# Expert routing in a fused attention, dense layer and mixture-of-experts kernel: choice, ranks and slot lists built in groups of four token tiles

## What is computed

```python
# 1. attention, 4 batches x 8 heads, 576 x 64, half the heads with a local mask, half with a strided one
attn = softmax(mask(q @ k.T / 8)) @ v
# 2. a dense layer, 512 -> 1024 -> 512
h = x @ w_in
solu = h * softmax(h)
x2 = (layer_norm(solu) * g_ln) @ w_out
# 3. top-1 mixture of 8 experts, 512 -> 1024 -> 512
logits = x2 @ w_gate + modality_bias[modality_id]
e_idx = argmax(logits, axis=1)                 # one expert per token
gate_w = softmax(logits)[arange(N), e_idx]
for e in range(8):
    mask = e_idx == e
    out[mask] = gate_w[mask, None] * (relu(x2[mask] @ w1[e]) @ w2[e])
```

## Time and profile before

| | us |
|---|---|
| median of 3 executions | 636.38 |
| lowest, highest | 634.66, 639.98 |
| the profiled execution, its own time | 635.12 |
| its span, first to last instruction | 633.4 |
| granted TensorE clock, mean | 0.995 |

### The profile page before, as it was taken

The page is one execution under the profiler, slowest core; times in us unless marked ns, Lnnn a source line. Parts: engine busy times, 40 slices in busy tenths (PEclk is TensorE's granted clock), DMA queues, the critical chain, the costliest instruction groups (busy, mean ns, idle before and its releaser), DMA issues.

```text
span 633.4 us, 12550 instructions
## 1 busy us (share of the span) xinstructions
PE 607.4 (96%) x3794; PEld 505.3 (80%) x3795; DVE 359.4 (57%) x1032; ACT 242.1 (38%) x775; POOL 205.6 (32%) x242
## 2 busy tenths in 40 slices
PE   4999999989999999999999998999999998999995
PEld 3677776768888888888888897998998976788994
DVE  5899999766787888888888954231211200021210
ACT  3788888824233333334344322212222211112210
POOL 5555555530333433455554434110011011101001
PEclk9999999999999999999999999999999998999999
DMA  8877667100000070000000000010870035000000
GB/s 184 177 170 166 159 161 176 49 0 18 18 32 18 17 283 17 17 33 17 17 17 17 18 34 1 31 37 21 303 275 17 31 120 215 17 15 31 0 30 33
DMA packets 70861, 47.35 MB, mean 75 GB/s; under 512 B 56728, under 2 KB 58744, under 8 KB 70832
## 3 DMA queue, kind: packets, MB, share of 16 engines
q1 hardware_dynamic: 68832, 41.21, 22.9%
q0 software_dynamic: 2000, 5.77, 2.5%
HBM read 37.40 MB, written 10.22 MB: 75 GB/s over the span
## 4 chain that ended last, share of the span: by engine, by line
PE 77%; issue 8%; POOL 7%; DMA 2%; DVE 2%; SPq 2%; ACT 1%; POOLq 0%; DVEq 0%; ACTq 0%
PE bank L571 16%; PE bank L997 16%; PE pair L982 16%; PE pair L571 15%; POOL work L543 4%; PE pair L1521 3%; PE pair L1090 2%; POOL w_lo L550 2%; PE pair L1511 2%; PE pair L1117 2%; PE bank L1110 1%; DMA xT<-x_dram,g_idx 1%; SPq L415 1%; DMA arena<-in_k 1%; PE pair L692 1%
## 5 line engine op out<-in xcount | busy, mean ns | idle before, releaser
L982 PE MATMUL pair<-x_hi,lead_hi 128*128 128x256 f32 x288 | 82.2, 285 | 0.2 <-DVE lead_h L1042 0.2
L982 PE MATMUL pair<-x_lo,lead_hi 128*128 128x256 f32 x288 | 81.5, 283 | 0.0
L982 PE MATMUL pair<-x_hi,lead_lo 128*128 128x256 f32 x288 | 81.5, 283 | 0.0
L1053 POOL DMA_INDIRECT out<-work,lead_sidx x18 | 18.0, 998 | 165.4 <-ACT work L1037 159.4
L763 ACT ACTIVATE work<-pair,neg_max 96x128 f32<-96x128 f32 (+2 forms) x176 | 61.6, 368 | 18.7 <-PE bank L703 14.8
L543 POOL TENSOR_TENSOR work<-work,row_inv 96x512 f32<-96x512 f32 (+3 forms) x48 | 44.8, 933 | 54.4 <-DVE row_inv L850 54.4
L1042 DVE SCALAR_TENSOR_TENSOR lead_h<-pair,lead_h 128x512 fp32r<-128x512 f32 x18 | 12.4, 691 | 86.7 <-ACT lead_h L1030 86.5
L1432 POOL TENSOR_TENSOR rstd<-ln_small 128x1 f32 (+1 forms) x18 | 26.5, 1472 | 107.2 <-DVE ln_small L638 107.2
L571 PE MATMUL bank<-w_hi,lnT_hi 128*128 128x512 f32 x144 | 58.5, 406 | 1.1 <-DVE lnT_lo L1269 1.1
L571 PE MATMUL pair<-w_hi,x_hi 128*128 128x512 f32 x144 | 58.3, 405 | 0.2 <-ACT arena L752 0.2
L571 PE MATMUL bank<-w_hi,lnT_lo 128*128 128x512 f32 x144 | 56.7, 393 | 0.0
(11 more groups left out here) (209 smaller groups left out, 1393.2 us busy)
## 6 DMA issues: line engine op xcount, KB each, us to landing
entry<-in_moe_w SPq DMA_DIRECT2D x12, 1024.0 KB, 9.3
arena<-in_q SPq DMA_DIRECT2D x32, 144.0 KB, 2.9
arena<-in_k SPq DMA_DIRECT2D x32, 144.0 KB, 3.4
x_dram<-work SPq DMA_DIRECT2D x18, 256.0 KB, 2.0
arena<-in_moe_w SPq DMA_DIRECT2D x8, 512.0 KB, 7.1
arena<-in_v SPq DMA_DIRECT2D x16, 144.0 KB, 2.6
work<-in_v SPq DMA_DIRECT2D x16, 135.0 KB
arena<-in_moe_w_in SPq DMA_DIRECT2D x8, 256.0 KB, 3.2
```

What stands on the lines that cost most here:

```text
L982: ins = pe.matmul(lead_h_ps[n % 2][:, jj * BLK:(jj + 1) * BLK], a[:, w], b[:, x], start=(passes == 1), stop=(passes == 3 * KC))
L1053: pool.indirect_dma_start(out=out, out_offset=bass.IndirectOffsetOnAxis(ap=lead_sidx[:, tt:tt + 1], axis=0), in_=lead_y[tt], in_offset=Non ...
```

## The change

The routing no longer runs tile by tile. The gate weights become the stationary operand: each of the four 128-row chunks of `w_gate` is padded with zeros to 32 columns and writes its partial logits to its own 32 rows of one PSUM bank, with up to 512 tokens (four tiles, `GROUPED`) moving. ScalarE copies the bank, TensorE transposes it back tile by tile, and one VectorE reduction adds the four partial sums. Group 0 (tiles 0 to 3) is done in slot 6, for the choice of the leader; groups 1 to 4 are all done in slots NT and NT+1. Choice, exponentials and gates are done for all tiles of a phase at once, and the ranks with two matmuls and a scan. The inverse is no longer a matmul: the rank gives a row of a table in DRAM, POOL writes (token, gate) pairs there with 18 indirect DMAs of 8 bytes per token, and SP's seven copies read from the table. The second copy of the transposed x2 (`x2_T`), `spread`, `invert_slots`, `add_slots` and the count matmul are gone. The slots end at NT+1.

```diff
-        wg = sb("wg", KC * E)
+        wg = sb("wg", KC * STRIDE)
...
+        slot_tab = nc.dram_tensor("slot_tab", [E * T, 2], F32)
...
@@ attention_sp, behind the four constant loads
+            sp.wait_ge(consts, 3)
+            sp.dma_start(slot_tab.rearrange("(p n) w -> p (n w)", p=P), zeros).then_inc(tab_zeroed, 16)
...
@@ attention_dve
+            dve.memset(wg[:, :], 0.0)
...
-        LAST = NT + 3
+        LAST = NT + 2
...
+        GROUPED = [range(g, min(g + SNAP, NT)) for g in range(0, NT, SNAP)]
...
@@ solu_pe
+            def gate_logits(g):
+                first, n = group_cols(g)
+                pe.wait_ge(x2T_kept, GROUPED[g][-1] + 1)
+                wait(pe, lgT_out, g)
+                if g == 1:
+                    pe.wait_ge(lead_chosen, 1)
                 for c in range(KC):
+                    rows = slice(c * STRIDE, (c + 1) * STRIDE)
+                    ins = pe.matmul(lgT_ps[rows, 0:n], wg[:, rows], xT[:, c * T + first:c * T + first + n],
+                                    start=True, stop=True, skip_group_check=True)
+                ins.then_inc(lgT_ready, 1)
+
+            def turn_logits(g):
+                pe.wait_ge(lgT_out, g + 1)
+                wait(pe, lg_taken, g)
+                for k in range(len(GROUPED[g])):
+                    ins = pe.transpose(lg_ps[:, k * P:(k + 1) * P], lgT[:, k * P:(k + 1) * P], ident[:, :])
+                ins.then_inc(lg_turned, 1)
...
+            def ranks():
+                pe.wait_ge(hot_ready, 2)
+                pe.matmul(lgT_ps[:, 0:NE], before[:, :], hot[:, :], start=True, stop=True)
+                pe.matmul(lgT_ps[:, NE:2 * NE], ones_bf[:, :], hot[:, :], start=True, stop=True,
+                          skip_group_check=True).then_inc(rank_ready, 1)
 
             def slot(t):
                 if at(t, NT):
                     lead_up(pe, 0, 0)
-                    ranks(t - 3)
+                    gate_logits(1)
                     turn_x2(t - 2)
                     turn_ln(t - 1)
                     lead_up(pe, 0, 1)
-                    logits(t - 2)
+                    turn_logits(1)
+                    gate_logits(2)
                     down(t - 1, 0)
-                    invert_slots(t - 3)
+                    turn_logits(2)
+                    gate_logits(3)
                     down(t - 1, 1)
                     return
                 if at(t, NT + 1):
                     lead_up(pe, 0, 2)
-                    ranks(t - 3)
+                    turn_logits(3)
                     turn_x2(t - 2)
                     lead_up(pe, 0, 3)
-                    logits(t - 2)
-                    return
-                if at(t, NT + 2):
-                    ranks(t - 3)
+                    gate_logits(4)
                     lead_down(pe, 0, 0)
-                    invert_slots(t - 4)
+                    turn_logits(4)
                     lead_down(pe, 0, 1)
-                    invert_slots(t - 3)
+                    ranks()
                     return
...
@@ solu_act
             def take_x2T(t):
                 act.wait_ge(x2_turned, t + 1)
-                wait(act, lg_ready, t)
-                act.copy(x2_T, x2T_ps[:, :]).then_inc(x2T_out, 1)
                 act.copy(xT[:, :]...
...
@@ solu_dve, behind the slots; place() is twelve small operations on 128x18 to 128x144 elements
             lead_rest_x(dve, 1, 1)
-            add_slots(NT - 2)
-            add_slots(NT - 1)
-            lead_block_dve(dve, 1)
+            gates(2, SNAP, NT)
+            for n in range(4):
+                lead_rest_h(dve, 1, n)
+            lead_stage_scatter(dve, 1)
+            place()
+            lead_rest_x(dve, 2, 0)
+            lead_rest_x(dve, 2, 1)
...
@@ solu_pool
             def slot(t):
-                if inside(t, 3):
-                    spread(pool, t - 3)
...
             lead_block_pool(pool, 0)
             lead_block_pool(pool, 1)
+
+            pool.wait_ge(tab_zeroed, 16)
+            pool.wait_ge(tab_idx_ready, 1)
+            for t in range(NT):
+                pause(pool)
+                pool.indirect_dma_start(out=slot_tab, out_offset=bass.IndirectOffsetOnAxis(ap=tab_idx[:, t:t + 1], axis=0),
+                                        in_=tok_pair[:, 2 * t:2 * t + 2], in_offset=None).then_inc(tab_written, 16)
...
@@ experts_sp
             sp.wait_ge(meta_ready, 1)
+            sp.wait_ge(tab_written, 16 * NT)
             with sp.Fori(0, E - 1) as k:
...
-                sp.dma_start(slots[:, :].rearrange("p (i n) -> p i n", i=2)[:, :, bass.ds(first, NT)],
-                             inv[:, 0:2 * E * NT].rearrange("p (i n) -> p i n", i=2)[:, :, bass.ds(e * NT, NT)]
-                             ).then_inc(slots_ready, 16)
+                sp.dma_start(slots[:, bass.ds(2 * first, 2 * NT)],
+                             slot_tab.rearrange("(e p n) w -> e p (n w)", e=E, p=P)[bass.ds(e, 1)]
+                             .rearrange("o p m -> (o p) m")).then_inc(slots_ready, 16)
```

More of the change, by code:

```diff
@@ L162, in fused_kernel @@
         first_w = sb("first_w", E)
[L163 to L177, removed]
+        iota_e = sb("iota_e", E)
+        NE = E * NT
+        rt = sb("rt", 5 * NE)
+        lgs, lg_exp, eq_w, run_n, rank_of = (rt[:, i * NE:(i + 1) * NE] for i in range(5))
+        by_te = lambda x: x.rearrange("p (t e) -> p t e", e=E)
+        by_et = lambda x: x.rearrange("p (e t) -> p e t", e=E)
+        hot = sb("hot", NE, BF16)
+        not_first = sb("not_first", NE)
+        tok_f = sb("tok_f", 5 * NT)
+        l_max, sum8, rank_f, row_base, rank_hi = (tok_f[:, i * NT:(i + 1) * NT] for i in range(5))
+        rank_i = sb("rank_i", 2 * NT, I32)
+        tab_idx = sb("tab_idx", NT, I32)
+        zeros = rt[:, 0:2 * E * T // P]
         n_f = sb("n_f", 2 * E)
@@ L895, in slots_of @@
                 body(t)
-            with eng.Fori(3, SNAP + 3) as t:
+            with eng.Fori(3, SNAP + 2) as t:
                 body(t)
-            for t in range(SNAP + 3, FIRST_PIECE):
+            for t in range(SNAP + 2, FIRST_PIECE):
                 body(t)
@@ new lines, in turn_logits, with count_snap @@
+            def turn_logits(g):
[4 more added lines that the diff above has]
+                ins.then_inc(lg_turned, 1)
+            def count_snap():
+                pe.wait_ge(hot_ready, 1)
+                pe.matmul(lgT_ps[:, 0:E * SNAP], ones_bf[:, :], by_et(hot[:, :])[:, :, 0:SNAP],
+                          start=True, stop=True).then_inc(snap_ready, 1)
@@ L1165, in slot @@
                     up_tile(pe, t, 0)
-                if inside(t, 3):
-                    ranks(t - 3)
+                if at(t, SNAP + 2):
+                    gate_logits(0)
+                if at(t, SNAP + 3):
+                    count_snap()
                 if inside(t, 2):
@@ L1171, in slot @@
                     turn_ln(t - 1)
+                if at(t, SNAP + 2):
+                    turn_logits(0)
                 if not (static(t) and t < 2):
                     up_tile(pe, t, 1)
-                if inside(t, 2):
-                    logits(t - 2)
                 if inside(t, 1):
                     down(t - 1, 0)
-                if inside(t, 3):
-                    invert_slots(t - 3)
-                if inside(t, 1):
                     down(t - 1, 1)
@@ L1330, in slot @@
                     lead_rest_h(dve, 0, 1)
+                    take_logits(1)
+                    take_logits(2)
                 if at(t, NT + 1):
+                    take_logits(3)
                     lead_rest_h(dve, 0, 3)
+                    take_logits(4)
+                    choose(2, SNAP, NT)
                 if inside(t, 0):
```

242 lines of the change are left out of this document (116 added, 126 removed).

## The result

The changed kernel takes 640.44 us (median of 20, 637.22 to 641.92) where the kernel before takes 636.75 (median of 20, 634.66 to 640.33). The ratio is 1.0048, with a 95% interval from 1.0031 to 1.0066: slower by half a per cent. The forecast was 620.0 with a range to 627.5, so it was wrong by 20 us and on the wrong side. The profiled execution has a span of 637.5 us, against 633.4.

What follows compares the result with a forecast made beforehand. TensorE, busy 96% of the span, was taken as the bound. From 635.12 us, 23.2 of removed work went and 7.6 of added came, making 619.5; half of 1.26 on top gave 620.0, range 615.0 to 627.5.

Steps and rivals of the forecast that it cites:

- The slot lists: POOL and SP queues: 18 indirect writes at 1.29 us each and seven copies, all hidden with 1.4 us slack.
- the sum: Whole kernel: 635.12 - 23.2 + 7.6 = 619.5 us, plus half of 1.26 gives 620.0.
- Rival 4: `turn(0)`, block 5: slot table too late; chance 0.08 still faster, 0.04 slower than before; 643.8 at 2.7 us each.
- Column groups: `gate_logits` on TensorE: four matmuls work at the same time, 1.06 us a full group, 0.63 the last, 4.9 together.
- Rivals 1 and 2: `gate_logits`: overlap only in part, 2.15 us a group, 625.8, chance 0.20; no overlap, 3.44, 631.6, chance 0.08.
- rival 1: `gate_logits`: records start in program order, so only neighbours overlap; 2.15 us a group, 625.8 in all; chance 0.20.
- turn_logits: Added on TensorE: 18 transposes back, at 0.49 us for four, 2.2 us together.
- ranks and counts: Added on TensorE: `ranks` and `count_snap` once, three small bf16 matmuls, 0.2 us.
- waits: TensorE's new waits for ScalarE's bank copies and VectorE's operations, mostly covered by other work: 0.3 us.
- At the start: Ahead of attention's loop: a small VectorE memset and one more DMA, taken as 0, upper bound 3.9 us.
- Is TensorE still last?: Solu slots: each shrinks by 1.18 to 12.37 us; low part of x keeps a slack of 0.45, so TensorE stays last.
- Rival 3: Solu slots: VectorE's chain sets the slot, each gives back some 0.2 us, 2.8 together, 622.8; chance 0.12.

Runs made afterwards that it cites:

- group 3: Changed kernel untouched, 622.74 us, and with three edits that do nearly nothing, 624.58, 622.69 and 622.63; the kernel before beside them, 635.34.
- the five groups: The sets in which all follow-up kernels ran, each on one chip at one time with its own runs of the kernel before; 622.63 to 656.28 us.
- both groups: Changed kernel without its 18 indirect writes, in two sets of runs: 623.03 us (ratio 0.9755) and 623.02 us (ratio 0.9782).
- the dummies of group 1: Kernel before plus 18 indirect DMAs behind block 1's scatters: 8-byte writes 637.21 us, 2 KB writes 638.12, 8-byte reads 637.51.
- the four variants of group 2: Changed kernel with writes to another table, 624.74 us; SP not waiting on the writes' semaphore, 623.22; writes a block later, 630.40; in three bunches, 637.11.

## Why the prediction was wrong

**The step that failed** is "The slot lists", where the 18 indirect writes were "all hidden". I priced them as time of POOL, and looked for their harm at the end of their chain. As a chain they did as forecast or better: in group 3 1.29 us each (forecast 1.29), seven copies and their waits from 435.61 to about 459 in group 3 (24 us, forecast 32.4), weights from 461.65. No engine but SP waited for it. The harm was beside them: on three of six occasions (the record and the five groups) TensorE and ScalarE nearly stop while they are issued. The earlier trace rows could not show it: in the trace of before indirect DMAs stand alone, in pairs or in threes, and about four in a row are free. And the 1.5 us more of POOL's closing DRAIN, which came on every occasion, stand in no term of the sum. Rival 4 named the writes, "An 8-byte row may cost POOL or the DMA engines more", but put the price on the wrong engines and the place at `turn(0)`. Its place was wrong by itself, too: the slots are first missed at 477 us by VectorE, with some 18 us of slack in group 3 (copies done by about 459).

**Most of the rest held.** In group 3 the untouched kernel took 622.74, and without its writes it took 623.0 in both groups: forecast 620.0, range to 627.5. Such times of different groups can't be compared to better than about 2 us: in the traces without a late start, block 1 of the changed kernel starts anywhere from 384 to 386.5.
- Column groups: 0.99 to 1.00 a full group and 0.57 the last, forecast 1.06 and 0.63. Rivals 1 and 2 are refuted: 2.15 or 3.44 a group would have shown. The Trainium skill, "TensorE: Matmul & The Clock Gate", Part 3, gives 2.38x for three column tiles; here four give 3.44/1.00 = 3.4x with both changes of shape counted in, so nearer the ideal than that. Its statement that matmuls start and end strictly in order may be true all the same: the consequence that I drew from it in rival 1 did not come.
- `turn_logits` 0.44 for four (0.49), ranks and counts 0.14 (0.2), waits none (0.3). All that was added comes to 4 x 1.00 + 0.57 + 18 x 0.11 + 0.14 = 6.7, forecast 7.6. At the start nothing was lost.
- "Is TensorE still last? It holds, narrowly" didn't quite. Rival 3 came, in the later half of the stage: the changed kernel's up projections stand 12.6 us apart from 260 us on, and 12.37 was forecast. The chain of waits of the changed kernel:

```profile
260.10 0.12 issue
260.23 2.99 PE pair L568 x12
...
272.74 0.12 issue
```

The record waits for the low part of x, as forecast for this rival ("every slot gives back some 0.2"): seven such slots at 0.27, and one of 12.9 (239.00 to 251.90), make 2.4. With the 0.9 by which the additions were cheaper, that accounts for 13.8 instead of 15.6, to 0.3 us, which is closer than executions agree. Group 3 measured 622.7 and rival 3 had said 622.8, but that is luck in part: rival 3 had priced the slots alone, at 2.8, and they made 2.4; what was added on TensorE cost 0.9 less, and the DRAIN 1.5 more.

So the forecast was some 3 us short in any event, by the slots of rival 3 and by the DRAIN. The 17 us are another matter: no reading of the trace of before would have given them, but the chance of 0.04 for "slower" said more than I could know of 18 back-to-back DMAs of a kind that this kernel never issued in a row.

**What stays open: the cause of the dry stretch.** Shown are four things. It needs the writes. Where it comes, it needs nothing else of the change. It came only where most completion records of the writes are missing. And it grows with the number of writes in a row. A reading that fits these is that the path on which engines report their events fills up. The Trainium skill, "NOTIFIC — the notification-queue block", The write path, says that this block holds back its producers rather than lose a record inside. The same page, Interfaces, names this backpressure, from a full queue or internal FIFO, as what can stall an engine. Its section Constraints, capacities, measured rates says that the block can hold about 500 records. Each write gives 16 completions, TensorE starts and ends a weight load and a matmul every 0.12 us, and some five us of both are free before the stall: that is 64 completions and some 84 instructions with two records each, together some 230 records, about half of those 500 if none drained (an estimate from that page and the rows above). Two things don't fit it by themselves: records did go missing, and POOL, which is recorded like the others, kept its 1.26 us from write to write through the dry stretch. No run here shows the block itself. It would mean that the stall belongs to executions that are recorded. All of those compared here are, each with a granted clock to its name, so whether the changed kernel stalls when nobody records can't be told from them. Why some occasions lose records and others don't stays open as well; the chip alone doesn't decide it.

## What to carry to other kernels

That POOL is idle doesn't make dense rows of small indirect DMAs free. Look at what the other engines do beside the first row of them, and count about four in a row as the most that this kernel showed harmless on the bad occasions. Put the untouched kernel beside every experiment on the same chip at the same time: the dummies of group 1 and the four variants of group 2 said nothing on the question that they were made for, because the dry stretch didn't come there. And when a chain is moved to idle queues, find its first reader by the waits in program order (here VectorE, ahead of block 5), not the one you think of.

## What the runs showed of the hardware that I had not expected

- While POOL issued more than about four indirect writes 1.26 us apart, on three of six occasions TensorE took one weight load per 0.7 us instead of 0.12 and ScalarE stood for 14 us, at a DMA busy share of 0.02. On the other occasions neither happened.
- The granted clock fell after the idle time: 0.74 in the window from 420 us, 0.50 in the next two, 0.55 from 435 to 440 with TensorE busy again, which added about 2.3 us to the records that followed.
- POOL's closing DRAIN took 3.59 us with 18 more indirect DMAs in the kernel, reads or writes, dense or spread, and 2.12 us without them.
- Four column groups of 32 in one float32 pass over 512 columns ran at the same time: 1.00 us for four matmuls that take 0.86 each alone.
- A memset on POOL with a semaphore wait behind it holds back the next indirect DMA by 0.81 us, where two DMAs in a row are 0.30 apart.
